# Attention stage: every product except the one with V moved to the two row halves of TensorE, with queries and keys laid out by feature

## What is computed

```
B, H, S, D = 4, 8, 576, 64
q_rot, k_rot = rotate(q), rotate(k)        # x1*cos - x2*sin, x1*sin + x2*cos over the halves of D
scores = (q_rot @ k_rot.T) / sqrt(D)
attn = exp(scores - max(scores)); attn = attn / (sum(attn) + 1e-9)
x = (attn @ v) as (B*S, H*D)               # 2304 x 512
x = (sigmoid(x @ w_gate) * (x @ w_val)) @ w_out                   # d_ff 1536
h = x @ w_in; solu = h * softmax(h); y = layernorm(solu) * g @ w_out2   # d_ff 1024
```

## Time and profile before

| | us |
|---|---|
| median of three runs (lowest, highest) | 950.04 (949.89, 950.26) |
| the profiled execution | 951.31 |
| its span | 949.5 |
| PE busy in the span | 940.8 (99%) |
| DVE, ACT, POOL busy in the span | 480.5, 366.9, 340.1 |

### The profile page before, as it was taken

How to read it: one execution, slowest core, us unless ns; L and a number is a source line. 1 busy time by engine, 2 the same in 40 slices (tenths; PEclk the granted TensorE clock), 3 DMA queues, 4 the chain that set the end, 5 groups by cost and what they waited for, 6 DMA issues and landing times.

```text
span 949.5 us, 15393 instructions
## 1 busy us (share of the span) xinstructions
PE 940.8 (99%) x5367; PEld 784.1 (83%) x5367; DVE 480.5 (51%) x862; ACT 366.9 (39%) x800; POOL 340.1 (36%) x246
## 2 busy tenths in 40 slices
PE   8999999999999999999999999999999999999998
PEld 6888878888877888888888888888888888888886
DVE  6888888878772333323323323233453564444441
ACT  6888888888762111111111111111111333333332
POOL 4656575665335606005004103202666322222200
PEclk9999999999999999999999999999999999999999
DMA  3434343433412200200100200100210011111111
GB/s 109 118 108 118 101 129 94 126 99 108 137 52 79 67 1 1 67 1 1 67 0 2 67 0 1 44 0 0 66 67 0 1 23 23 22 22 22 22 22 44
DMA packets 37890, 48.21 MB, mean 51 GB/s; under 512 B 8416, under 2 KB 24288, under 8 KB 37856
## 3 DMA queue, kind: packets, MB, share of 16 engines
q1 hardware_dynamic: 37632, 47.47, 17.8%
q10 hardware_dynamic: 224, 0.28, 0.1%
...
## 4 chain that ended last, share of the span: by engine, by line
PE 96%; ACT 2%; issue 1%; POOL 0%; DVE 0%; POOLq 0%; DVEq 0%; ACTq 0%
PE ps L1189 31%; PE ps L1234 16%; PE ps L1297 10%; PE ps L1129 9%; PE ps L1171 9%; PE ps L1272 9%; PE ps L1153 8%; PE ps L1098 2%; PE ps L1282 2%; PE ps L1061 1%; ACT prob L765 0%; POOL x_lo L728 0%; ACT kT L831 0%; ACT kT L825 0%; ACT qT L820 0%
## 5 line engine op out<-in xcount | busy, mean ns | idle before, releaser
L1189 PE MATMUL ps<-x_hi,w_hi 128*128 128x512 f32 (+1 forms) x480 | 177.0, 369 | 0.0
L1189 PE MATMUL ps<-x_lo,w_hi 128*128 128x512 f32 (+1 forms) x480 | 176.7, 368 | 0.0
L1189 PE MATMUL ps<-x_hi,w_lo 128*128 128x512 f32 (+1 forms) x480 | 176.6, 368 | 0.0
L990 DVE TENSOR_TENSOR hid<-ps,sig 128x512 f32<-128x512 f32 (+1 forms) x60 | 38.3, 638 | 241.8 <-PE ps L1189 210.1
L797 ACT ACTIVATE sig<-ps 128x512 f32<-128x512 f32 (+1 forms) x60 | 33.3, 555 | 299.2 <-PE ps L1189 299.2
L923 DVE TENSOR_REDUCE nmax<-ps 128x1 f32<-128x576 f32 x144 | 108.3, 754 | 45.8 <-PE ps L1129 45.4
L1129 PE MATMUL ps<-kT,qT 128*128 128x288 f32 x640 | 120.9, 315 | 2.7 <-ACT prob L765 1.4
L667 POOL TENSOR_SCALAR w_hi<-raw_w 128x1024 fp32r<-128x1024 f32 x15 | 41.2, 2772 | 215.5 <-PE ps L1234 215.5
L1129 PEld LDWEIGHTS ps<-kT,qT 128*128 128x128 f32 x640 | 89.8, 189 | 18.5 <-ACT prob L765 10.4
L1189 PEld LDWEIGHTS ps<-x_hi,w_hi 128*128 128x128 f32 x480 | 90.5, 189 | 15.4 <-issue 0.5
L1189 PEld LDWEIGHTS ps<-x_hi,w_lo 128*128 128x128 f32 x480 | 90.5, 189 | 15.2
...
## 6 DMA issues: line engine op xcount, KB each, us to landing
kT<-kT SPq DMA_DIRECT2D x30, 304.0 KB, 4.3
...
```

The lines of the kernel that those rows point to most:

```text
L1189: last = nc.tensor.matmul(in_parts(gv_ps[f][n][:, 0:size(c)], c), w, x, start=m == 0, stop=m == len(todo) - 1)
```

## The change

- The host lays queries and keys out by feature: for each pair and head a block of 64 features by tokens, with a copy rolled by 32 features next to it. Rotation is then one product with a table that holds cos and sin, in place, and one sum of the two copies. It stays on POOL (`RQ`, `RK`), and the lower pieces of the pair ahead (`ql`, `kl`) go to POOL as well. No transposes of queries and keys are left on PE; ACT rounds `rot_q` and `rot_k` in one operation each (`qh`, `kh`).
- Partitions 0 to 63 hold one half of the keys and 64 to 127 the other. A score tile is three products (hi\*hi, lo\*hi, hi\*lo), each as two matmuls with 64 rows, one for each half of the array, that write different banks. `T` on SP copies the query pieces to the other partitions (`q_twice`, four transfers a pair).
- The transposes take blocks of 64 rows by 128 columns, two for each block of before, into two banks. `A` and `B` of one index are one item `AB`, and its halves are copied out as `x` and `y`. `TQ`, `KT` and `RT` are one item `Q`. Ahead of each turn PE increments a semaphore (`pe_holds`). `flip` in the last stage is changed the same way.
- `PV0` is run in three parts (`PV0a`, `PV0b`, `PV0`) among the score tiles. V is laid out by the host too and takes three transfers instead of six. The output rows are no longer strided.
- The first pair is rotated on DVE and POOL in two parts, and its scores begin when the first part is there.

The core of the diff:

```diff
-        ORDER_PE = ["A2", "S0", "A3", "K", "S1", "RT", "B1", "B3", "k", "S2", "KT", "T", "S3", "PV0", "S4", "TQ",
-                    "B0", "q", "S5", "A0", "S6", "PV1", "S7", "B2", "S8", "A1"]
...
-        ORDER_POOL = ["RK", "RQ", "XL"]
...
+        ORDER_PE = ["Q", "S0", "S1", "K", "AB2", "S2", "PV0a", "S3", "AB0", "S4", "PV0b", "AB3", "S5", "S6", "PV0", "AB1", "S7", "S8", "PV1"]
+        ORDER_ACT = ["qh", "Qx", "Qy", "S0", "S1", "AB2x", "S2", "AB0x", "S3", "S4", "AB3x", "S5", "S6", "AB3y", "kh", "S7", "S8", "AB1x"]
+        ORDER_DVE = ["S0", "Kx", "S1", "Ky", "S2", "AB2y", "S3", "S4", "AB0y", "S5", "S6", "PV0", "S7", "S8", "AB1y", "INV", "PV1"]
+        ORDER_POOL = ["ql", "RQ", "kl", "XL", "RK"]
+        ORDER_SP = ["LQ", "RW", "RR", "T", "LK", "LV"]
+        FIRST_PE = ["S0", "S1", "S2", "S3", "AB0", "S4", "S5", "S6", "AB1", "S7", "S8"]
+        FIRST_ACT = ["kB", "S0", "qB", "S1", "S2", "AB0x", "S3", "S4", "S5", "qh", "S6", "kh", "S7", "S8", "AB1x"]
+        FIRST_DVE = ["S0", "kB", "qB", "S1", "S2", "S3", "S4", "AB0y", "S5", "S6", "S7", "S8", "AB1y", "INV"]
...
+        LAST_PE = ["Q", "K", "AB2", "AB3", "PV0a", "PV0b", "PV0", "PV1"]
+        LAST_ACT = ["Qx", "Qy", "AB2x", "AB3x", "AB3y"]
+        LAST_DVE = ["Kx", "Ky", "AB2y", "PV0", "PV1"]
+        WARM = 16
+        FILL = {"S0": 1, "S1": 1, "S2": 1, "S3": 1, "S4": 1, "S5": 1}
+        BETWEEN = {"AB3": (0,), "PV0": (1, 2), "PV1": (3,)}
+        AHEAD = {"AB2": -1, "AB3": -1, "K": -1, "Q": -1, "PV0a": -1, "PV0b": -1, "PV0": -1, "PV1": -1, "XL": -1, "RW": -1, "RR": -1, "qh": 1, "kh": 1, "ql": 1, "kl": 1, "T": 1, "RQ": 2, "RK": 2, "LK": 2, "LQ": 2}
+        ITEMS = [n for n in ORDER_PE if n[:2] == "AB" or n in ("K", "Q")]
...
+        def p_parts(name, r, src, u):
...
+            if name == "Q":
+                return [(pT[u][:, :, r * S + MAIN:r * S + S], half.rearrange("p (k n) -> p k n", k=MT)),
+                        (rinv_t[:, quarter], src[0:SLOTS, 2 * P + TAIL:3 * P]),
+                        (pK[u][ROWS[r], MAIN:S], src[ROWS[r], 2 * P:2 * P + TAIL])]
+            col = int(name[2]) * P + r * D
+            heads = pT[u][:].rearrange("p k (h n) -> p h k n", h=2)
+            return [(heads[:, :, :, col:col + D], src.rearrange("p (h k n) -> p h k n", h=2, k=MT))]
+
...
+        def q_column(j, r):
+
+            if j == 2 * MT:
+                return ((S, SIDE + MAIN), (SIDE + S, MAIN))[r]
+            i, h = j // 2, j % 2
+            return (0 if i // 2 == r else SIDE) + h * QM + i % 2 * P
+
...
+            def twice_q(p, halves=range(2)):
+
+                sp.wait_ge(q_lo, num(p) + 1)
+                for x in q_pieces[par(p)]:
+                    for r in halves:
+                        sp.dma_start(x[ROWS[r], SIDE:SIDE + WIDE].bitcast(F32), x[ROWS[1 - r], 0:WIDE].bitcast(F32)
+                                     ).then_inc(q_twice, 16)
...
+            def rotate(p, raw, arrived, products, prod, lo_done, rot, done):
+
+                pool.wait_ge(arrived, num(p) * 16)
+                for dst, tab in products:
+                    last = nc.gpsimd.tensor_tensor(dst, dst, tab, ALU.mult)
+                last.then_inc(prod, 1)
+                pool.wait_ge(prod, num(p))
+                pool.wait_ge(lo_done, num(p))
+                nc.gpsimd.tensor_tensor(rot[:], raw[:, 0, :], raw[:, 1, :], ALU.add).then_inc(done, 1)
+
+            q_products = [(raw_q[:, :, 0:MAIN].rearrange("p c (h n) -> p c h n", h=2), twice(tab_q[:, :, 0:QM])),
+                          (raw_q[:, :, S:], tab_q[:, :, QM:])]
+            k_products = [(raw_k[:, :, TAIL:].rearrange("p c (h n) -> p c h n", h=2), twice(tab_k[:, :, 0:SH])),
+                          (raw_k[:, :, 0:TAIL], tab_k[:, :, SH:])]
+
...
+            def rest(p, piece, rot, hi_done, lo_done):
+
+                pool.wait_ge(hi_done, num(p) + 1)
+                nc.gpsimd.tensor_tensor(piece[1], rot, piece[0].bitcast(F32), ALU.subtract).then_inc(lo_done, 1)
 
...
+            def piece_hi(p, pieces, rot, rotated, done):
+
+                act.wait_ge(rotated, num(p) + 1)
+                if not early(p, 2):
+                    act.wait_ge(sc_full, num(p) * SLOTS - SLOTS)
+                nc.scalar.activation(pieces[par(p)][0][:, 0:WIDE], rot[:], ACT.Copy).then_inc(done, 1)
...
+                if item == "Q" and not early(p, 1):
+                    act.wait_ge(x_norm[1], num(p))
+                for n, (dst, part) in enumerate(p_parts(item, r, tr_ps[bank], par(p))):
                     last = nc.scalar.activation(dst, part, ACT.Copy)
+                    if item == "Q" and n == 1:
+                        last.then_inc(turned_inverses, 1)
                 last.then_inc(tr_out[bank], 1)
...
-                tail = 2 * MAIN
-                half, both = S // 2, (kT[u], kTs[u])
-                if j < 2 * MT:
-                    h = j % 2
-                    q0 = h * MAIN + j // 2 * P
-                    todo = [[(q0, k_[:, h * S + b * half:h * S + (b + 1) * half], 0) for k_ in both] for b in range(2)]
-                else:
-                    todo = [[(tail, k_[:, b * half:(b + 1) * half], 0) for k_ in both] for b in range(2)]
-                    b_main, zero_b = S + TAIL, tail + TAIL
-                    for b in range(2):
-                        todo[b] += [(zero_b, k_[:, b_main + b * half:b_main + (b + 1) * half], 0) for k_ in both]
-                for b in range(2):
-                    for n, (q0, keys, c0) in enumerate(todo[b]):
-                        c0 += b * half
-                        last = nc.tensor.matmul(dst[:, c0:c0 + keys.shape[-1]], qT[u][:, q0:q0 + P], keys, start=n == 0,
-                                                stop=n == len(todo[b]) - 1)
+                (qh, ql), (kh, kl) = q_pieces[u], k_pieces[u]
+                todo = []
+                for x, y in ((qh, kh), (ql, kh), (qh, kl)):
+                    if j < 2 * MT:
+                        todo.append((x, [q_column(j, r) for r in range(2)], y, (SH + TAIL, 0)[j % 2]))
+                    else:
+                        todo += [(x, [q_column(j, r)[h] for r in range(2)], y, (SH + TAIL, TAIL)[h]) for h in range(2)]
+                for n, (x, q0, y, k0) in enumerate(todo):
+                    for r in range(2):
+                        last = nc.tensor.matmul(dst[:, r * SH:(r + 1) * SH], x[ROWS[r], q0[r]:q0[r] + P], y[ROWS[r], k0:k0 + SH],
+                                                start=n == 0, stop=n == len(todo) - 1)
                 last.then_inc(sc_full, 1)
...
+                pe.sem_inc(pe_holds, 1)
...
+                    blocks = [prob[int(name[2])][:, c + t * P:c + (t + 1) * P] for c in (0, S + TAIL) for t in range(MT)]
+                for b, block in enumerate(blocks):
+                    for r in range(2):
+                        src = block if block is not None else prob_t[:, MAIN:MAIN + NARROW] if r == 0 else prob_t[:, MAIN - TAIL:S]
+                        last = nc.tensor.transpose(tr_ps[banks[r]][0:src.shape[-1], b * D:(b + 1) * D], src[ROWS[r], :],
+                                                   eye_f[ROWS[r], ROWS[r]])
+                        if b == len(blocks) - 1:
+                            last.then_inc(tr_full[banks[r]], 1)
+
+            def pv(n, p, part):
...
+            PARTS = {"PV0a": slice(0, 4), "PV0b": slice(4, 6), "PV0": slice(6, 10), "PV1": slice(0, 10)}
...
                 for kk in range(KT2):
-                    last = nc.tensor.transpose(lt_ps[:, kk * P:(kk + 1) * P], ln[u][:, kk * P:(kk + 1) * P], eye_f)
+                    for r in range(2):
+                        last = nc.tensor.transpose(ps[:, 4 + r, kk * D:(kk + 1) * D], ln[u][ROWS[r], kk * P:(kk + 1) * P],
+                                                   eye_f[ROWS[r], ROWS[r]])
                 last.then_inc(lt_full, 1)
```

More of the change, by code:

```diff
@@ L306, in newest @@
             steps = {}
-            for n in names:
-                back = -AHEAD.get(n, 0)
+            for n in [(name, r) for name in names for r in range(2)]:
+                back = -AHEAD.get(n[0], 0)
                 steps[BANK[n]] = max(steps.get(BANK[n], (-9, 0, n)), (back, RING.index(n), n))
@@ L492, in swap @@
[L492 to L500 removed]
+                    sp.dma_start(dst[ROWS[h], 2 * MT + h, :], tails[h]).then_inc(v_in[par(p)], 16)
@@ L747, in _ @@
         def _(act):
-            def qk_hi(name, p, step):
-                bank, before = use(name, step)
-                act.wait_ge(tr_full[bank], before + 1)
-                for dst, src, rows in hi_parts(name, tr_ps[bank], par(p), kT):
-                    last = nc.scalar.activation(dst[rows], src[rows], ACT.Copy)
-                last.then_inc({"q": q_hi, "k": k_hi, "T": t_hi}[name], 1)
+            def piece_hi(p, pieces, rot, rotated, done):
[3 more added lines that the diff above has]
+                nc.scalar.activation(pieces[par(p)][0][:, 0:WIDE], rot[:], ACT.Copy).then_inc(done, 1)
             def exps(j, p):
@@ L926, in turned @@
             def turned(name, p, step):
```

(36 more changed lines are left out.)

560 lines of the change are left out of this document (237 added, 323 removed).

## The result

The changed kernel takes **945.17 us** (median of 12 runs, 940.76 to 948.46) against 950.26 for the kernel before on the same chip (12 runs; one of them, 4841.70, stands apart and hardly moves the median): ratio 0.9946, 95% interval 0.9929 to 0.9964. It is faster by 0.5%; 916 was forecast, with a range of 896 to 939. The profiled run took 945.95, with a span of 944.2 and a mean clock of 0.978, where before had 1.00.

What follows compares the result with a forecast made beforehand. PE was taken to bound attention, ACT and DVE close behind. Savings of 24.6 (steps), 9 (start) and 2 (last stage), less 1.5 (end of attention), make 34.1: 917.2 profiled, given as 916, range 896 to 939.

Steps and rivals of the forecast that it cites:

- start: First pair, without transposes and swaps ahead: `S0` at 8.5 us, step 0 ending near 21 for 30; 9 us saved.
- 14 steps: Steady attention: each step falls from 16.76 to 15.0 us, 24.6 us saved over 14.
- end of attention: Last pair into the gate: `XL` waits for `PV1` behind `S8`, so the first `w_lo` comes late; 1.5 us lost.
- last stage: `flip` as eight half-block pairs, 0.77 us with switches and hold; 18 x 0.11, 2 us saved.
- hand schedule: One attention step traced across the engines, ACT's `Qx` waiting for `x_norm[1]`: 15.0 us, PE 89% busy.
- The clock: Sign for the start: a clock fall between the first two score tiles would make the start wrong; no size given.
- The loop: Score tiles wait for exponentials two tiles back: 2.38 us for two tiles, within a step of 15.0.
- A pair of half blocks: PE price of two half-row transposes side by side: 0.07 us, between bounds of 0.055 and 0.132.
- the rival of 0.132: Half blocks as dear to issue as to compute: step 16.0, `flip` loses 6.5 us, 938 in all; chance 20%.
- Overlap better than by hand: ACT's wait ahead of `Qx` is covered, only PE and POOL bind: step 13.8, 898 us; chance 16%.

Runs made afterwards that it cites:

- the fastest kernel: Changed kernel with V load first, ACT's `Qx` wait moved, first pair and second `k_lo` on DVE, retuned zero products at start, more in last step: 926.18 us.
- zeros set anew: Changed kernel with V load first, ACT's `Qx` wait moved, first pair and second `k_lo` on DVE, start's zero-product batches retuned: 929.94 us.
- only the first ones: Changed kernel with V load first, ACT's `Qx` wait moved, first pair on DVE, zero products at start but none behind `S8` and `Q`: 932.16 us.

## Why the prediction was wrong

By its own steps, from the chain pieces (before: 39.18, 273.77, 294.27, end 949.5; after: 52.59, 269.31, 289.71, 944.2):

| stretch | forecast | measured | missed by |
|---|---|---|---|
| start, to the first `PV1` | -6.0 | +13.4 | 19.4 |
| 14 steps | -24.6 | -17.9 | 6.7 |
| end of attention, `PV1` to `PV1` | -1.4 | -0.1 | 1.3 |
| last stage | -2 | -0.7 | 1.3 |

The forecast's own figures for the two ends were -9 and +1.5, read at other places. Its "for 30" was the first `RT`, 30.20, ahead of which two score tiles of the second pair had already run; the first pair's last tile was through at 27.2, so a step 0 that ends at 21 saves 6.1 and not 9. And `PV1` stood ahead of `S7` and `S8` before and stands behind `S8` now: from 21, by the hand schedule's 15.0 less a `PV1` of 2.85, the first one comes at 33.2, 6.0 before 39.18, and at the end the two tiles fall out of the stretch: from a `PV1` to the first gate product it took 9.2 before, and 7.8 was forecast, `w_lo` late and all. The sum stays as it was, 34, since the two shifts cancel by luck; the table has the forecast at the places that were measured.

- **Start: the step that failed.** "`S0` at 8.5, `S1` near 12 ... so step 0 ends near 21" put the work of DVE and POOL side by side at the prices that each has alone, with loads "to 4.3 as before". The first pair's last tile was through at 33.6, 12.6 late, and from there the first `PV1` took another 6.8 more than forecast. Four things stood against it.
  1. DVE and POOL hold each other up: 2.54 and 2.73 us for what takes 0.95 and 0.56 with POOL still, and the latter 0.56 too where it starts 0.34 ahead of POOL's. The first pair on DVE gave 5.0 us, its new order included. The Trainium skill has the rule, "SBUF — State Buffer", "SBUF: two separate sides": a DVE operation with two inputs in SBUF and a GpSimd operation that reads SBUF take one pair of ports by turns, each for its whole length. The traces agree: `q_lo` ended 0.41 us behind POOL's operation, 0.15 less than its lone 0.56; the rule was not weighed.
  2. The clock: while operands were late PE ran at 0.50; holding it gave 4.1 us with the operands at the same places. Over the 12 runs of the changed kernel, too, a mean clock of 0.980 or 0.981 went with 940.76 to 941.69, and 0.972 with 947.6 to 948.09, though the slowest, 948.46, had 0.974. The forecast named this as what would make the start wrong, but gave it no price.
  3. The second pair: the sum let step 1 follow at once at 21, but POOL's row for it takes 16.4 us and starts only when its queries have landed, at 18.38 (19.39 in the changed kernel). Moving one operation off it did not free the tile, since the copies of the queries hang on the same row. It still stands in the best kernels: with DVE, clock and zeros mended the first pair's last tile is through at 26.2 and the second pair's first one starts at 33.01, and the first `PV1` is at 44.60 (46.84 in the fastest kernel), against 39.18 before. This is the largest part that is left, and only the traces show it; no run took it away.
  4. Loads: POOL's first product had its queries at 8.16, not near 4.3. It is worth little: in the kernel with the V load first they came 1.37 earlier, `S0` 1.28, and the first `PV1` 0.63.
- **The loop: right.** The hand schedule's 15.0 and its reason, ACT behind `x_norm[1]`, were borne out by the row of 1.13 us and by 14.55 once the wait was gone. A pair of half blocks, 0.07 by forecast, takes 0.065, and the rival of 0.132 is out. *Overlap better than by hand* (13.8) did not come, even without that wait.
- **14 steps: 11 were right**, at 14.93 to 15.13. One took 16.68: behind gaps of 0.63 and 0.77 us PE's clock was 0.72 and 0.85 (88 to 96 us). The gaps do not explain it: the step at 144 has 0.63 and 0.78 in the same places, and its clock stayed at 1.00. The thirteenth and fourteenth took 34.98 for 29.9: 3.53 us of waiting for V, then the low clock. The forecast multiplied one step by 14 and passed over an edit in `step_in`: before, only two weight loads went ahead of V and the third behind it, and nothing waited; now all three go ahead. That, not the half rows, is what the 5 us are, since V first takes them away.
- **End of attention: right up to the gate.** The first gate product comes 7.85 behind the start of the last `PV1` ahead of it (269.24 to 277.09), the forecast's 7.8. In the changed kernel gaps of 1.20, 0.53 and 0.88 us ahead of the transposes fill that time; with zeros in them PE comes there earlier and waits 0.40 for `w_lo`, as forecast, and the product again stands at 7.84. What was missed is the clock behind it: most of the first twelve gate products start 0.43 apart in place of 0.23, and the last step is 20.40, where it is 18.7 to 18.8 at 1.00.
- **Last stage: a size.** Forecast 0.11 for each of 18, measured 0.3 to 0.5 in all against whole blocks. From the start of the product ahead to the first follower it is 0.96 (786.11 to 787.07): eight pairs take 0.64, less than the 0.79 of whole blocks, but 0.32 passes before the first, where other items follow each other in 0.23. The rest of the 0.74 between the two kernels is not accounted for.
- **Sum.** 19.4 + 6.7 + 1.3 + 1.3 = 28.7, the miss between 917.2 and 945.95.

Open: which runs dip, and where. Steps of 16.6 to 16.7 stand in four of the six profiles with the wait on `x_norm[1]`, one or two in each, and in none of the six without it (PE 94.6% busy against 91.5% in the 160 us from 60 to 220), which fits denser work, but two with it have none either and no run isolates it. And why the two kernels with the zeros set anew or only the first ones stayed 2 us over their expected medians.
